# A fused attention and two-expert kernel: the experts' steps start four slots later beside the attention, and the opening is reordered

## The chip, the cores and the metric

The kernel runs on 1 core of a Trainium2 chip. The metric is the device time of one execution in microseconds (us); lower is better. The kernel before takes 1138.91 us (median of 3 runs, 1137.67 to 1141.26).

Five engines run their own instruction lists in order and meet only at semaphores: PE (TensorE, matrix products and transposes), DVE (VectorE), ACT (ScalarE), POOL (GpSimd), and SP (SyncE), which here only issues DMAs. "An engine waits" means that its next instruction stands at a semaphore and everything behind it stands too.

## The reference, cut to what matters

```python
# attention: B=4, H=8, S=768, D=40; state is D x D for each (b, h)
for t in range(S):
    y[:, :, t] = einsum('bhd,bhde->bhe', r_t, state)
    Sa = einsum('bhde,bhe->bhd', state, a_t)
    state = state * w_t[..., None, :] - Sa (x) b_t + v_t (x) k_t
x = y as rows: 3072 tokens x 320
# first expert: d_ff 1024
h = ((x @ w1) * (x @ w2)) @ w3
x2 = h @ w_out
# second expert: d_ff 2048
out = maximum(x2 @ w_in, 0)**2 @ w_out2
```

Everything is float32. The products of the experts are taken from operands split into a rounded part and its rest ("hi" and "lo"), three products for each.

## The kernel before, in words

**Attention.** The sequence is cut into chunks of 64 tokens; a *window* n is one chunk of half of the batch, 24 windows in all (`WINDOWS`), windows with even n for one half of the batch and odd n for the other. A window is a chain of small steps over all engines: `turn_w`, `turn_ar`, `turn_bk` (transposes of loaded rows, PE), `scan` (running decay, DVE), `cross` (PE), `mask_ak` and `fill_lanes` (DVE), `invert` (POOL: 62 dependent operations that invert a 32x32 triangular block in all lanes at once), `turn_inverse` (DVE: brings the inverse into place), `make_u0`, `make_x1`, `make_u1`, `turn_uv`, `add_state`, `make_read`, `make_y`, `turn_state` (PE), with copies on ACT between them. At the end `scale_y` (DVE) writes y, `store_y` (SP) stores it to DRAM (`xT`).

**Experts.** The tokens are cut into 6 *tiles* (`TILES`) of 512, and tile i needs the y of windows 4i to 4i+3: `load_x` (SP) brings them back from DRAM, `round_x` (ACT) makes `xT_hi`, `rest_x` (DVE) makes `xT_lo`. A tile is 56 *steps* (each a `yield` of the generator `experts()` that every engine has): steps 0 to 23 are the first expert (a_f and b_f, products of 8 matmuls into `aside`, L848, and `fold`, L901), steps 24 to 55 are the second (c_f, L848, alternating with `project`, L916, here called p_f). `round_x` of the next tile stands in step 54 on ACT, `rest_x` in step 54 on DVE; steps 52 to 55 are c15, p13, p14, p15.

**Folding and splitting.** w3 and w_out of the first expert are multiplied once, in 8 parts (`turn_w3`, `multiply_w3` on PE, `round_fold` on ACT, `rest_of_fold` on DVE, `store_fold` on SP into `fold_rows`). The other weights are split into hi and lo once: the raw weights are loaded into one of 3 `stage` buffers (`load_staged`), `round_split` and `rest_of_split` make the parts in a slot of `w_ring` or `v_ring`, `pass_split` on SP stores them and issues the load of the split three further on. These splits stand beside tile 0, each in a step of its own (`slot_of_w`, `due`), those below zero before it.

**Order.** It is written out by hand, the same on each engine. First the *opening*: windows 0 to 3 whole, the first part of window 4 (up to `make_z(4)`), the first part of window 5 (up to `cross(5)`), the folding, and splits 0 to 2. Then the *loop*: for n from 4 to 23, 14 slots a window; in each slot every engine does a piece of window n (or n+1, n+2) and then `next(beside)`, one step of the experts. So windows 4 to 23 stand beside 280 steps, that is tiles 0 to 4, and tile 5 (56 steps) runs alone after the attention. Before, step t stands in slot t: the 14 slots of window 4 have steps 0 to 13, and each tile begins with the first slot of window 8, 12, 16 or 20. On PE the slots of window n are, in order: `turn_ar(n+1)` s0, `make_z(n)` s1, `turn_bk(n+1)` s2, `cross(n+1)` s3, s4, `make_u0(n)` s5, `turn_rows(n+1)` s6, `make_x1(n)` s7, `turn_w(n+2)` `make_u1(n)` s8, `turn_uv(n)` s9, `add_state(n)` s10, `make_read(n)` s11, `make_y(n)` s12, `turn_state(n)` s13, where s0 to s13 are the expert steps. For n = 4 the first four of these attention pieces are left out on PE, since the opening has done them. `turn_ar(n+1)` waits for `st_copied`, which is `copy_state` on ACT, and that stands on ACT behind step s12.

Of the kernel before, what the change touches and what calls it, by code (L numbers as in the profile page):

```python
# [5 lines left out]
F32 = mybir.dt.float32  # L6
# [71 lines left out]
def attention_with_experts(nc, xT_dram, inputs, w1, w2, w3, w_out, w_in, w_out2, out):  # L78
# [8 lines left out]
    T, M = out.shape  # L87
# [4 lines left out]
    DX = M + REM  # L92
    FT, FT2 = F // P, F2 // P
# [5 lines left out]
    W_FIRST, V_FIRST = FT + FT2 // 2, FT + FT2  # L99

    OPENING = 4
    LEAD = 0
    LOOK = 3
    assert REM * 2 == P and TOK == B * 2 * C and STAGE >= 2 * DX

# [8 lines left out]
    with ExitStack() as ctx:  # L114
# [94 lines left out]
        def wait(eng, s, value):  # L209
            if value > 0:  # L210
                eng.wait_ge(s, value)
# [74 lines left out]
        def turning(u):  # L286
            return banks[2 + u % 2]

        def folding(ft):
            return banks[4 + ft % 2][:, 0:M]  # L290


        def slot_of_w(at):
            return max(3 * at - 7, -1) if at < FT else 19 if at == FT else 17 + 4 * (at - FT)

        splits = sorted([(slot_of_w(at), 0, at) for at in range(W_FIRST)] +
                        [(23 + 2 * f, 1, FT + f) for f in range(FT2)])
# [6 lines left out]
        for x in range(FT + len(splits)):  # L304
            before = staged_count[x - LOOK] if x >= LOOK else 0
            staged_count.append(before + 16 * (1 if x < FT or splits[x - FT][1] else 6))

        def wait_fold_stored(eng):
            for x in range(RING):
                eng.wait_ge(fold_stored[x], 64 * len(range(x, FT, RING)))  # L310


        clears = [azk[0], rbd[0], azk[1], rbd[1], *spare, *zv, *sT, *st]
# [20 lines left out]
        def _(sp):  # L334
            def begin(loads):
                for signal, buffer, src in loads:
                    sp.dma_start(buffer, src).then_inc(signal, 16)
# [25 lines left out]
            def load_wo():  # L363
                for h in range(2):
                    rows = w_out[GT // 2 * P * h:GT // 2 * P * (h + 1), :].rearrange("(t p) m -> p t m", p=P)
                    sp.dma_start(wo_raw[h][:].rearrange("p (t m) -> p t m", m=M), rows).then_inc(loaded_wo, 16)
# [18 lines left out]

            def store_fold(ft):
                sp.wait_ge(fold_split, ft + 1)
                for rest, t in enumerate((h_hi, h_lo)):
                    row, src = fold_rows[ft][:, DX * rest:DX * (rest + 1)], t[ft % RING][:, 0:M].bitcast(F32)
                    sp.dma_start(row[:, 0:M], src).then_inc(fold_stored[ft % RING], 16)  # L390
                    sp.dma_start(row[:, M:DX], src[:, 2 * P:M]).then_inc(fold_stored[ft % RING], 16)

# [30 lines left out]
            def load_v(at):  # L423
                x = at % V_FIRST
                if x < FT:
                    sp.wait_ge(fold_stored[x % RING], 64 * (x // RING + 1))
                if V_FIRST <= at < V_FIRST + SLOTS:
                    sp.wait_ge(v_stored[at % SLOTS], 16 * (FT2 // SLOTS))
                wait(sp, h_used, at - SLOTS + 1)
                dst = v_ring[at % SLOTS][:].bitcast(F32)  # L430
                if x < FT:
                    sp.dma_start(dst, fold_rows[x]).then_inc(v_loaded[at % SLOTS], 16)
                else:
                    sp.dma_start(dst[:, 0:2 * M], wout_rows[x - FT]).then_inc(v_loaded[at % SLOTS], 16)
# [3 lines left out]
            def pass_split(x):  # L438
                store_split(x)
                if x + LOOK < len(splits):  # L440
                    load_staged(FT + x + LOOK)
# [5 lines left out]
                    yield  # L447

            def experts():
                w_at = v_at = SLOTS  # L450
                for i in range(TILES):
                    for f in range(FT + LAG):
                        if f < FT:
                            yield
                            if W_FIRST <= w_at < W_LOADS:
                                load_w(w_at)
                            w_at += 1
                            yield
                        if f >= LAG:
                            if v_at < FT or V_FIRST <= v_at < V_LOADS:  # L460
                                load_v(v_at)
                            v_at += 1
                            yield
                    for f in range(FT2 + LAG):
                        if f < FT2:
                            if f % 2:
                                if W_FIRST <= w_at < W_LOADS:
                                    load_w(w_at)
                                w_at += 1
                            yield  # L470
                        if f >= LAG:
                            if v_at < FT or V_FIRST <= v_at < V_LOADS:
                                load_v(v_at)
                            v_at += 1
                            if f < FT2 + LAG - 1:
                                yield
                    wait_drained(sp, f"o{SUB - 1}", i)
                    wait_drained(sp, f"o{SUB - 2}", i)
                    wait_drained(sp, "o0", i)
                    wait_drained(sp, "o1", i)  # L480
                    sp.dma_start(out.rearrange("(b s) m -> s b m", b=B)[2 * C * i:2 * C * (i + 1)],
                                 out_rows[:]).then_inc(out_stored, 16)
                    yield

            beside = split_first()
            def next_w(n):
                sp.wait_ge(turned_w, n)
                begin(inputs.w_loads(n))

            def next_ar(n):  # L490
                sp.wait_ge(turned_ar, n)
                begin(inputs.ar_loads(n))

            def next_bk(n):
                sp.wait_ge(turned_bk, n)
                begin(inputs.bk_loads(n))
# [14 lines left out]
            begin(inputs.ar_loads(0))  # L511
            begin(inputs.bk_loads(0))
            load_staged(0)
            begin(inputs.uv_loads(0))
            next_w(1)
            load_wo()
            next_ar(1)
            load_staged(1)
            next_bk(1)
            sp.wait_ge(cleared, len(clears))  # L520
            begin(inputs.zv_loads(0))
            begin(inputs.zv_loads(1))
            next_w(2)
            load_staged(2)
            next_ar(2)
            begin(inputs.uv_loads(1))
# [31 lines left out]
            next_zv(5)  # L558
            store_fold(5)
            store_y(2)  # L560
            load_x(0, 0)
            store_y(3)
            load_x(0, 1)
            pass_split(0)
            store_fold(6)
            next_staged(10)
            pass_split(1)
            load_v(0)
            load_v(1)
            store_fold(7)  # L570
            load_v(2)
            load_v(3)
            pass_split(2)
            next_uv(5)
            beside = split_first()
            for n in range(OPENING, WINDOWS):
                one, two = window_steps(n)
# [87 lines left out]
        def _(pe):  # L665
# [255 lines left out]
                last.then_inc(h_used, 1)  # L921

            def experts():
                pe.wait_ge(y_scaled, OPENING)
                pe.wait_ge(st_copied, OPENING)
                for i in range(TILES):
# [37 lines left out]
            cross(0)  # L964
            turn_w(1)
            turn_rows(0)
            multiply_w3(0, 0)
            make_z(0)
            turn_ar(1)
            multiply_w3(0, 1)  # L970
            multiply_w3(0, 2)
            turn_bk(1)
# [135 lines left out]
        def _(act):  # L1108
# [66 lines left out]
            def round_fold(ft):  # L1175
                act.wait_ge(multiplied, ft + 1)
                wait(act, fold_stored[ft % RING], 64 * (ft // RING))
                nc.scalar.copy(h_hi[ft % RING][:, 0:M], folding(ft)).then_inc(fold_rounded, 1)

            def round_split(x):  # L1180
                _, kind, at = splits[x]
# [8 lines left out]
            def round_hidden(x, i):  # L1190
                at = (FT + FT2) * i + x
                wait_made(act, x, i)
                if at == 0:
                    wait_fold_stored(act)
                wait(act, h_used, at + 1 - RING)
                nc.scalar.copy(h_hi[at % RING][:], hidden[x % 2][:]).then_inc(hi_made, 1)  # L1196

# [16 lines left out]
                nc.scalar.copy(xT_hi[:], x_raw[:]).then_inc(x_rounded, 1)  # L1214

            def experts():
                act.wait_ge(multiplied, FT)
                for i in range(TILES):
                    for f in range(FT + LAG):
# [106 lines left out]
            copy_w3(7)  # L1326
            round_x(0)
            round_fold(7)
            round_split(2)
            for n in range(OPENING, WINDOWS):  # L1330
                one, two = window_steps(n)
                if OPENING < n and one:
# [32 lines left out]
        def _(dve):  # L1365
# [97 lines left out]

            def rest_of_fold(ft):
                dve.wait_ge(fold_rounded, ft + 1)
                nc.vector.tensor_tensor(h_lo[ft % RING][:, 0:M], folding(ft), h_hi[ft % RING][:, 0:M].bitcast(F32),
                                        ALU.subtract).then_inc(fold_split, 1)

            def rest_of_split(x):
# [34 lines left out]
                nc.vector.tensor_tensor(xT_lo[:], x_raw[:], xT_hi[:].bitcast(F32), ALU.subtract).then_inc(x_split, 1)  # L1504

            def experts():
                for i in range(TILES):
                    for f in range(FT + LAG):
                        if f < FT:
# [89 lines left out]
            invert_decay(4, 0)  # L1599
            new_state(1)  # L1600
            scale_a(4)
            turn_inverse(2)
            invert_decay(4, 1)
            mask_read(1)
            scale_bk(4)
            rest_of_fold(4)
            scale_y(1)
            mask_ak(4)
# [3 lines left out]
            add_x1(2)  # L1612
            invert_decay(5, 1)
            rest_of_split(0)
            turn_inverse(3)
            rest_of_fold(5)
            new_state(2)
            rest_of_split(1)
            mask_read(2)
            add_x1(3)  # L1620
# [6 lines left out]
            scale_bk(5)  # L1627
            rest_x(0)
            rest_of_fold(7)
            rest_of_split(2)  # L1630
            for n in range(OPENING, WINDOWS):
                one, two = window_steps(n)
                if OPENING < n and one:
# [65 lines left out]
```

## Time and profile before

| | |
|---|---|
| median of 3 runs | 1138.91 us |
| profiled execution | 1141.75 us |
| its span (first to last instruction) | 1139.3 us |
| PE busy | 1065.8 us, 94% of the span |
| POOL, DVE, ACT busy | 559.7, 634.3, 411.3 us |
| mean granted TensorE clock | 0.969 of full |
| moved by DMA | 172.74 MB, mean 152 GB/s |

Span and execution differ by 2.45 us, which lie around the span. The page of the profile cuts the span into 40 slices of 28.5 us and gives the busy share of each engine in tenths, and the clock that TensorE was granted. An engine's idle time is listed before the instruction that ended it, with the releaser.

### The profile page before, as it was taken

How to read it: one execution, taken by the hardware profiler on the slowest of the kernel's cores; microseconds unless marked ns; L12 is line 12 of the kernel's file. 1: busy time of each engine (PE TensorE's matmuls, PEld its weight loads, DVE VectorE, ACT ScalarE, POOL GpSimd, SP SyncE). 2: the span in 40 equal slices, each digit the busy share in tenths (PEclk: the TensorE clock that was granted, in tenths of full speed). 3: DMA queues.
4: the chain of work that ended last, by engine and by line, in shares of the span. 5: the costliest groups of instructions: out<-in, count | busy, mean ns of one | idle time of the engine just before them, and what ended most of it. 6: DMA issues, size and time to landing. Idle time of an engine off the chain costs nothing.

```text
span 1139.3 us, 27869 instructions
## 1 busy us (share of the span) xinstructions
PE 1065.8 (94%) x11056; PEld 903.7 (79%) x11056; DVE 634.3 (56%) x987; ACT 411.3 (36%) x771; POOL 559.7 (49%) x1573
## 2 busy tenths in 40 slices
PE   4997879999979999989999998999998999988998
PEld 4776757888867888877888986888886888876897
DVE  5866336677745566646466655566565556332343
ACT  2443323444433244323244333234333234322232
POOL 5778707367554374573464672554662654700000
PEclk9998889999989999998999998999998999998999
DMA  9943277666866546655545656546555453454552
GB/s 182 178 91 79 62 218 204 149 179 201 225 189 150 147 132 162 155 159 139 153 129 149 146 167 149 146 131 151 149 162 145 139 153 120 127 167 160 167 173 81
DMA packets 269504, 172.74 MB, mean 152 GB/s; under 512 B 201792, under 2 KB 231488, under 8 KB 269376
## 3 DMA queue, kind: packets, MB, share of 16 engines
q1 hardware_dynamic: 269376, 170.97, 57.0%
q8 instruction: 88, 1.44, 0.5%
q14 instruction: 40, 0.33, 0.1%
HBM read 144.18 MB, written 26.74 MB: 150 GB/s over the span
## 4 chain that ended last, share of the span: by engine, by line
PE 74%; DVE 3%; DMA 2%; issue 2%; SPq 2%; ACT 1%; DVEq 0%; ACTq 0%
PE aside L848 30%; PE moe_bank L916 13%; PE moe_bank L901 9%; PE both L810 3%; PE both L711 3%; PE both L752 2%; PE both L744 2%; PE both L825 2%; PE both L821 2%; PE both L695 2%; PE both L793 2%; PE both L724 1%; PE both L705 1%; PE both L801 1%; PE both L775 1%
## 5 line engine op out<-in xcount | busy, mean ns | idle before, releaser
L650 POOL TENSOR_TENSOR inv_tmp<-blk,inv 128x60 f32<-128x60 f32 (+24 forms) x744 | 253.0, 340 | 261.1 <-DVE blk L1419 204.1
L654 POOL TENSOR_TENSOR inv<-inv,inv_tmp 128x60 f32<-128x60 f32 (+24 forms) x744 | 263.7, 354 | 58.2
L916 PE MATMUL moe_bank<-v_ring,h_hi 128*128 128x320 f32 x768 | 178.5, 320 | 0.0
L848 PE MATMUL aside<-xT_hi,w_ring 128*128 128x512 f32 x480 | 143.0, 430 | 16.7 <-DVE xT_lo L1504 7.2
L1499 DVE TENSOR_TENSOR hidden<-left 128x512 f32<-128x512 f32 x96 | 68.0, 708 | 129.6 <-ACT left L1208 129.6
L1196 ACT CAST h_hi<-hidden 128x512 fp32r<-128x512 f32 x144 | 89.5, 621 | 124.6 <-DVE hidden L1495 78.9
L848 PE MATMUL aside<-x2T_hi,w_ring 128*128 128x512 f32 x480 | 132.7, 406 | 0.0
L916 PEld LDWEIGHTS moe_bank<-v_ring,h_hi 128*128 128x128 f32 x768 | 127.3, 189 | 3.8
L1487 DVE TENSOR_TENSOR h_lo<-hidden,h_hi 128x512 fp32r<-128x512 f32 x144 | 99.3, 690 | 51.4 <-ACT h_hi L1196 50.6
L1208 ACT ACTIVATE left<-aside 128x512 f32<-128x512 f32 x96 | 57.3, 597 | 178.8 <-PE aside L848 113.0
L848 PEld LDWEIGHTS aside<-xT_hi,w_ring 128*128 128x128 f32 x480 | 90.5, 201 | 36.0 <-DVE xT_lo L1504 7.5
L916 PE MATMUL moe_bank<-v_ring,h_lo 128*128 128x320 f32 x384 | 119.0, 310 | 0.0
L848 PEld LDWEIGHTS aside<-x2T_hi,w_ring 128*128 128x128 f32 x480 | 84.0, 188 | 14.9 <-ACT x2T_hi L1232 0.2
L901 PE MATMUL moe_bank<-h_hi,v_ring 128*128 128x512 f32 x288 | 92.8, 403 | 0.0
L848 PE MATMUL aside<-xT_lo,w_ring 128*128 128x512 f32 x288 | 86.1, 409 | 0.0
L1377 DVE RECIPROCAL undecay<-decay 104x256 f32<-104x256 f32 x48 | 83.7, 1745 | 0.5
L848 PE MATMUL aside<-x2T_lo,w_ring 128*128 128x512 f32 x288 | 81.5, 391 | 0.0
L916 PEld LDWEIGHTS moe_bank<-v_ring,h_lo 128*128 128x128 f32 x384 | 72.5, 189 | 0.0
L1495 DVE TENSOR_TENSOR hidden<-left,aside 128x512 f32<-128x512 f32 x48 | 32.5, 676 | 69.7 <-PE aside L848 69.7
L848 PEld LDWEIGHTS aside<-xT_lo,w_ring 128*128 128x128 f32 x288 | 57.7, 200 | 13.4
L635 POOL MEMSET azk<- 64x512 f32 x20 | 10.4, 522 | 109.8 <-PE both L744 109.6
L848 PEld LDWEIGHTS aside<-x2T_lo,w_ring 128*128 128x128 f32 x288 | 54.1, 188 | 12.2 <-DVE x2T_lo L1521 0.2
(144 smaller groups left out, 1628.1 us busy)
## 6 DMA issues: line engine op xcount, KB each, us to landing
w_ring<-gate_rows SPq DMA_DIRECT2D x40, 640.0 KB, 4.0
w_ring<-win_rows SPq DMA_DIRECT2D x40, 640.0 KB, 4.0
v_ring<-wout_rows SPq DMA_DIRECT2D x80, 320.0 KB, 3.0
v_ring<-fold_rows SPq DMA_DIRECT2D x48, 384.0 KB, 3.3
gate_rows<-w_ring SPq DMA_DIRECT2D x8, 640.0 KB, 4.1
win_rows<-w_ring SPq DMA_DIRECT2D x8, 640.0 KB, 3.6
wout_rows<-v_ring SPq DMA_DIRECT2D x16, 320.0 KB, 3.4
stage<-in_moe_w SPq DMA_DIRECT2D x8, 512.0 KB, 4.8
```

Source lines behind the costliest of these rows:

```text
L650: nc.gpsimd.tensor_tensor(tmp, x[:, j, 0:j].unsqueeze(2).broadcast_to([P, j, X - lo]), mine[:, j:j + 1, lo:X].broadcast_to([P, j, X - lo]) ...
L654: nc.gpsimd.tensor_tensor(mine[:, 0:j, lo:X], mine[:, 0:j, lo:X], tmp, ALU.add).then_inc(solve, 1)
L711: last = nc.tensor.matmul(its_both(n)[:, x * P:(x + 1) * P], bkT[n % 2][0:E, x].rearrange("e z s -> e (z s)"), azk[n % 2][0:E, x].rearrang ...
L810: last = nc.tensor.matmul(its_both(n)[:, x * P:(x + 1) * P], uvT[0:E, x, :], rbd_of(n)[0:E, x].rearrange("e q t -> e (q t)"), start=True, ...
L848: last = nc.tensor.matmul(bank(use), w, x, start=n == 0, stop=n == len(terms) - 1)
L901: last = nc.tensor.matmul(bank(f"x{m}"), weights[:, lo:lo + P], h[at % RING][:], start=f == 0 and n == 0, stop=f == FT - 1 and n == 2)
L916: last = nc.tensor.matmul(bank(f"o{s}")[:, 0:M], h[at % RING][:, s * P:(s + 1) * P], weights[:, rest * M:(rest + 1) * M], start=f == 0 and ...
L1196: nc.scalar.copy(h_hi[at % RING][:], hidden[x % 2][:]).then_inc(hi_made, 1)
L1208: drain(nc.scalar.activation(left[x % 2][:], bank(use), ACT.Relu), use)
L1377: nc.vector.reciprocal(undecay[0:E, xs], decay[n % 4][0:E, xs, 1:C + 1]).then_inc(undecayed, 1)
L1487: nc.vector.tensor_tensor(h_lo[at % RING][:], hidden[x % 2][:], h_hi[at % RING][:].bitcast(F32), ALU.subtract).then_inc(lo_made, 1)
L1499: nc.vector.tensor_tensor(hidden[x % 2][:], left[x % 2][:], left[x % 2][:], ALU.mult).then_inc(squared, 1)
```

## The change

The constant `LEAD` goes from 0 to 4. Each engine's `experts()` yields four times before its first step, so step t stands in slot t+4: slots 0 to 3 of the loop (window 4) hold no expert step, each later tile begins in slot s4 of window 8, 12, 16 or 20, and 60 steps run after the attention. `due` subtracts `LEAD`, so splits keep their step. The split of a2's weights goes from the opening to step 0.

The opening is reordered on SP, PE and DVE, `turn_inverse(2)` and `turn_inverse(3)` stand later on DVE, and the parts 6 and 7 of the folding are rounded and split in slots 2 and 3 of `v_ring` and no longer in `h_hi`/`h_lo`, so the first roundings of the experts wait for the stores of parts 0 to 5 only, and `load_v(2)`, `load_v(3)` wait for the stores of 6 and 7.

```diff
-    LEAD = 0
+    LEAD = 4
...
+        def folded(ft, rest):
+            if ft < 2 * RING:
+                return (h_hi, h_lo)[rest][ft % RING][:, 0:M]
+            return v_ring[SLOTS - FT + ft][:, M * rest:M * (rest + 1)]
...
-            return max(3 * at - 7, -1) if at < FT else 19 if at == FT else 17 + 4 * (at - FT)
+            return max(3 * at - 7, -1 if at < 2 else 0) if at < FT else 19 if at == FT else 17 + 4 * (at - FT)
...   (SP, load_v)
+                if SLOTS - FT + 2 * RING <= at < SLOTS:
+                    ft = FT - SLOTS + at
+                    sp.wait_ge(fold_stored[ft % RING], 64 * (ft // RING + 1))
...   (experts() of SP, PE, ACT and DVE)
+                for _ in range(LEAD):
+                    yield
...   (SP, opening)
             load_staged(0)
-            begin(inputs.uv_loads(0))
             next_w(1)
-            load_wo()
-            next_ar(1)
-            load_staged(1)
-            next_bk(1)
             sp.wait_ge(cleared, len(clears))
             begin(inputs.zv_loads(0))
+            next_ar(1)
+            load_wo()
+            next_bk(1)
+            load_staged(1)
             begin(inputs.zv_loads(1))
             next_w(2)
+            begin(inputs.uv_loads(0))
             load_staged(2)
...
             store_y(2)
+            pass_split(0)
             load_x(0, 0)
+            pass_split(1)
             store_y(3)
             load_x(0, 1)
-            pass_split(0)
+            next_staged(10)
             store_fold(6)
-            next_staged(10)
-            pass_split(1)
             load_v(0)
             load_v(1)
             store_fold(7)
+            next_uv(5)
             load_v(2)
             load_v(3)
-            pass_split(2)
-            next_uv(5)
...   (PE, opening)
-            multiply_w3(0, 0)
             make_z(0)
             turn_ar(1)
+            multiply_w3(0, 0)
...   (ACT)
-                nc.scalar.copy(h_hi[ft % RING][:, 0:M], folding(ft)).then_inc(fold_rounded, 1)
+                nc.scalar.copy(folded(ft, 0), folding(ft)).then_inc(fold_rounded, 1)
...
-                if at == 0:
-                    wait_fold_stored(act)
+                if at < RING:
+                    act.wait_ge(fold_stored[at], 64 * 2)
...
             round_fold(7)
-            round_split(2)
...   (DVE, opening)
             scale_a(4)
-            turn_inverse(2)
             invert_decay(4, 1)
             mask_read(1)
             scale_bk(4)
+            turn_inverse(2)
             rest_of_fold(4)
...
             rest_of_split(0)
-            turn_inverse(3)
             rest_of_fold(5)
             new_state(2)
+            turn_inverse(3)
             rest_of_split(1)
...
             rest_of_fold(7)
-            rest_of_split(2)
```

`store_fold` and `rest_of_fold` use `folded` in the same way.

## Rows read from the trace of the kernel before

**Rows 1.** The page: busy us (share of the span) xinstructions of each engine.
```profile
PE 1065.8 (94%) x11056; PEld 903.7 (79%) x11056; DVE 634.3 (56%) x987; ACT 411.3 (36%) x771; POOL 559.7 (49%) x1573
```

**Rows 2.** Timeline (start us, us, what [idle before <- releaser]), PE after the tile seams.
```profile
339.26 1.92 PE L695 MATMUL both<-ident,ar_raw 128*104 128x128 f32 x8 [4.85 <-ACT st L1166]
...
531.71 1.43 PE L848 MATMUL aside<-xT_hi,w_ring 128*128 128x512 f32 x5 [0.52 <-DVE hidden L1495]
...
862.18 1.92 PE L695 MATMUL both<-ident,ar_raw 128*104 128x128 f32 x8 [4.79 <-ACT st L1166]
```

**Rows 3.** The chain in order of time (start us, us, what), seam before tile 2.
```profile
504.07 0.70 DVE y_out L1461
...
509.56 2.33 DMA x_raw<-xT
...
513.29 0.43 ACT st L1166
```

**Rows 4.** Windows: us; busy of PE, PEld, DVE, ACT, POOL; PEclk, DMA share, GB/s.
```profile
513.90:518.80 4.90, 4.90 (x16) 3.96 (x16) 4.87 (x6) 1.62 (x4) 0.00 (x0) 0.50 0.05 18
...
150.00:180.00 30.00, 21.84 (x100) 16.02 (x99) 12.72 (x20) 8.89 (x17) 5.59 (x17) 0.77 0.81 215
```

**Rows 5.** The chain: pieces at full clock, and the end of the attention.
```profile
202.72 0.87 PE both L695 x8
203.59 1.84 PE aside L848 x8
205.43 1.06 PE both L744 x32
...
211.48 1.79 PE both L711 x16
...
493.91 1.76 PE moe_bank L916 x12
...
1017.69 1.05 PE both L825 x32
```

**Rows 6.** Timeline of PE: start of tile 0, late tile 0, start of tile 5.
```profile
150.63 1.40 PE L848 MATMUL aside<-xT_hi,w_ring 128*128 128x512 f32 x5
...
180.12 0.76 PE L775 MATMUL both<-uv,n 32*32 32x40 f32 x32
...
317.01 1.51 PE L793 MATMUL both<-ident,uv 128*104 128x128 f32 x8 [2.77 <-DVE decay L1369]
...
1029.65 2.50 PE L848 MATMUL aside<-xT_hi,w_ring 128*128 128x512 f32 x5 [7.22 <-DVE xT_lo L1504]
```

**Rows 7.** Timeline of ACT at the start of tile 0.
```profile
156.66 0.83 ACT L1188 CAST w_ring<-stage 128x768 fp32r<-128x768 f32 x1 [5.41 <-DMA stage<-in_moe_w]
...
165.94 0.62 ACT L1196 CAST h_hi<-hidden 128x512 fp32r<-128x512 f32 x1 [7.97 <-DMA fold_rows<-h_lo]
```

**Rows 8.** Timeline of SP (start us, us of issuing, what), end of the opening.
```profile
127.31 1.57 SPq L346 DMA_DIRECT2D xT<-y_out  x4
...
139.23 1.95 SPq L346 DMA_DIRECT2D xT<-y_out  x4
...
144.65 0.59 SPq L403 DMA_DIRECT2D gate_rows<-w_ring  x1
```

**Rows 9.** Timeline of PE and POOL in the opening.
```profile
95.13 1.93 PE L821 MATMUL aside<-rbd,st 40*40 40x64 f32 x32 [5.96 <-DVE ruv L1453]
...
117.57 0.76 PE L752 MATMUL aside<-x_row,invT 32*32 32x40 f32 x32 [2.55 <-DVE invT L1425]
...
116.61 0.20 POOL L654 TENSOR_TENSOR inv<-inv,inv_tmp 128x8 f32<-128x8 f32 x1
```

**Rows 10.** Timeline: DVE from `mask_ak` to `fill_lanes`; POOL's first solve in the loop.
```profile
526.86 0.86 DVE L1406 COPY diag<-both 32x256 f32<-32x256 f32 x2 [1.81 <-PE both L711]
...
529.07 2.01 DVE L1419 STREAM_TRANSPOSE blk<-diag 128x1024 f32<-128x1024 f32 x1
...
173.16 0.25 POOL L650 TENSOR_TENSOR inv_tmp<-blk,inv 128x31 f32<-128x31 f32 x1 [30.31 <-DVE blk L1419]
```

More of the change, by code:

```diff
@@ L306, in attention_with_experts @@
             staged_count.append(before + 16 * (1 if x < FT or splits[x - FT][1] else 6))
-        def wait_fold_stored(eng):
-            for x in range(RING):
-                eng.wait_ge(fold_stored[x], 64 * len(range(x, FT, RING)))
         clears = [azk[0], rbd[0], azk[1], rbd[1], *spare, *zv, *sT, *st]
@@ L387, in store_fold @@
                 sp.wait_ge(fold_split, ft + 1)
-                for rest, t in enumerate((h_hi, h_lo)):
-                    row, src = fold_rows[ft][:, DX * rest:DX * (rest + 1)], t[ft % RING][:, 0:M].bitcast(F32)
+                for rest in range(2):
+                    row, src = fold_rows[ft][:, DX * rest:DX * (rest + 1)], folded(ft, rest).bitcast(F32)
                     sp.dma_start(row[:, 0:M], src).then_inc(fold_stored[ft % RING], 16)
@@ L923, in experts @@
             def experts():
+                for _ in range(LEAD):
+                    yield
                 pe.wait_ge(y_scaled, OPENING)
@@ L1216, in experts @@
             def experts():
+                for _ in range(LEAD):
+                    yield
                 act.wait_ge(multiplied, FT)
@@ L1465, in rest_of_fold @@
                 dve.wait_ge(fold_rounded, ft + 1)
-                nc.vector.tensor_tensor(h_lo[ft % RING][:, 0:M], folding(ft), h_hi[ft % RING][:, 0:M].bitcast(F32),
+                nc.vector.tensor_tensor(folded(ft, 1), folding(ft), folded(ft, 0).bitcast(F32),
                                         ALU.subtract).then_inc(fold_split, 1)
@@ L1506, in experts @@
             def experts():
+                for _ in range(LEAD):
+                    yield
                 for i in range(TILES):
```

## The prediction

> **What bounds the kernel now.** I read the page first: PE is busy for 1065.8 of 1139.3 us and the next engine for little more than half of the span [rows 1]. So no engine but PE is a bound over the whole, and a change can gain only what PE stands idle (73.5 us) and what it loses at the lower clock. No product is taken away. Then I listed PE's idle times in order of time. They lie in four places: the opening, the start of tile 0, once at each tile seam, and before tile 5. Between two seams, 174 us apart (862.18 less 339.26, by three [rows 2]), PE has hardly a gap, so what the change does to the steady part is worth nothing unless it makes new gaps.
>
> A seam, in the chain of waits [rows 3]: the last `make_y` before it ends, `scale_y` starts at 504.07, y goes to DRAM and comes back as x_raw at 511.89, 7.8 us after `make_y`. ACT stands at `round_x` in step 54 for all that time, since step 54 is the very slot in which y is made. Behind it stands `copy_state`, which ends at 513.72, and `turn_ar` on PE waits for that: 4.85 us idle at the first seam, 4.79 at the last of four [rows 2]. After the gap PE gets half the clock (granted 0.50, that is 1.2 of 2.4 GHz) for 4.9 us [rows 4], so it loses another 2.4. Each seam costs 7.3 us. Before tile 5 the same trip costs 7.22 idle [rows 6], and a slow stretch of the same kind after it, 2.4: 9.6.
>
> The start of tile 0: from the first a0 at 150.63 to the end of `fold(0)` at 180.12 [rows 6]. In it are six products into `aside` at 1.84 (11.0), one `fold` (9 matmuls for 8: 2.1), `make_u0` and `turn_rows`, which I set at the 0.87 of `turn_ar` (1.7) [rows 5]: 14.8 us of work in 29.5. So 14.7 are lost, to two waits of ACT [rows 7], 5.41 for the raw weights of split 2 and 7.97 for the stores of fold parts 6 and 7, which the buffers of the first rounded hidden rows share, and to the clock (0.77 in the mean over these 30 us [rows 4]).
>
> **The change part by part.**
>
> *Four slots of lead, at the seams.* It adds and removes no instruction. `round_x` of the next tile moves from slot s12 to s2 of the next window. Counted on PE from the end of `make_y` with the pieces of [rows 5]: c14 1.84, `turn_state` (as `turn_ar`) 0.87, p12 1.76, `turn_ar` 0.87, c15 1.84, `make_z` 1.06: 8.2, after which ACT has a copy and a rounding before `round_x`, which it reaches at some 9 (estimate), and x is there at 7.8. `copy_state` and `turn_ar` are now ahead of it in ACT's list. The first a0 comes after p13, `turn_bk` (as `turn_ar`), p14, `cross` 1.79 and p15 more, at 16.2; `xT_lo` is ready at about 9 + 3.1 = 12.1 (tile 5 starts 10.9 after the end of the last `make_y` [rows 5, 6]; less the trip's 7.8 that leaves 3.1 for the two roundings). So 4 us of cover are left, and the seam is free: 4 x 7.3 = 29.2. The price below that: should x come 4 us later than now, a0 waits, no longer `turn_ar`. In each tile a wait of 0.52 for `combine`, queued behind `fill_lanes` on DVE [rows 2, 10], falls in slots where a1 and b1 stood; b1 now stands in s7, away from `fill_lanes` (s3): four of these, 2.0 less, and I count 1.5.
>
> *Before tile 5.* Behind the last `make_y` (ends 1018.74) two steps stood; now six: 2 x 1.84 + 4 x 1.76 = 10.7. The trip to `xT_lo` ends 10.9 after `make_y` [rows 5, 6]. Of 9.6 us 0.3 stay: 9.3 gained. The four steps that are now alone after the attention cost what they cost beside it, since both take PE in turn.
>
> *The uncovered slots 0 to 3.* On PE they hold nothing for window 4, so nothing is exposed there but `make_u0(4)`, which stood behind five steps and now stands behind one. It waits for `mask_ak(5)`; DVE gets there only after `rest_of_fold(7)`, whose product ends just before a0 starts at 150.6 (some 1.2 us for ACT's and DVE's part), `turn_inverse(4)` (0.7, both estimates) and 2.2 us of masking (526.86 to 529.07 [rows 10]): 154.7, and a0 from 150.6 ends at 152.5. So 2.2 us of idle. Below it: 0, if a0 itself is later; above: 6, if ACT's `copy_blocks(5)` is late too. POOL's inversion of window 5, which waited 30.3 us until 173.16 [rows 10], starts some 16 us sooner and is no bound.
>
> *The two waits at the start of tile 0.* The load for split 2 now goes out ahead of `store_fold(6)` and stands in no engine's way until step 0; the first rounding waits for parts 0 and 3 only, stored long before. Both waits go (above: one of them stays with 3 us). What is late next is x itself. SP has 10.3 us free between `store_y(2)` and `store_y(3)` (128.9 to 139.2 [rows 8]); into it go `load_x(0,0)` (four issues as `store_y`'s, 2.0 [rows 8]) and now two `pass_split`, each 7 issues of 0.59 (4.1) [rows 8]: 10.2, and waits between them, so `store_y(3)` goes out 0.2 to 1 us later, and I give a0 2 us of delay in all, with a slow stretch of 2.4 behind it. With the wait at `make_u0(4)`, partly inside it, 6 us of loss stay: 14.7 - 6 = 8.7 gained (3 to 13).
>
> Here a rule of the Trainium skill speaks against the change: "DMA: Bandwidth & Descriptors", section "Two DMAs through the same engine are not ordered", says that within one queue of one engine descriptors start in order, so y(3) would stand behind the 1.28 MB that the second `pass_split` has just sent. No run here shows that yet. At the 215 GB/s of [rows 4] these last 6.0 us, most of which have gone by when y(3) is issued: 1.5 us more by the rule, none without it. Both are inside the term's bounds.
>
> *The opening's order.* `zv_loads(0)` ahead of 1.8 MB lets `make_z(0)` go up to 5 us sooner; DVE's `turn_inverse(2)` no longer holds `mask_read(1)`, which takes away 5.96 us at 95.13; the slow 1.93 beside it goes too [rows 9]. But `make_u0(3)` at 117.57 waits for the inverse, and POOL, which does one solve after the other, ends that one at 116.81 [rows 9]. POOL's first solve starts from `fill_lanes(0)`, whose loads and predecessors are not touched. So all that PE wins before goes into a longer wait there. Behind it I count 1 us, for `new_state(2)` ahead of `turn_inverse(3)` (below: 2 us lost by a longer slow stretch after a longer gap; above: 4, if that slow stretch gets shorter).
>
> *Late in tile 0* PE waits 2.77 at 317.01 [rows 6], and runs slowly after it, as a split's load came late from an SP queue full with window 7's transfers. This burst now meets an earlier step, when loads of 6 DMAs still go out. Between 4 us gained and 6 lost I take 0.
>
> The sum: 29.2 + 1.5 + 9.3 + 8.7 + 1.0 + 0 = 49.7. Against it I set 3.5 us for waits that no row shows: the steps of the first expert meet the attention's pieces in another phase in each tile. That leaves 46.2. Against the profiled execution (span 1139.3, and 2.45 around it, 1141.75) this is 1095.6; the median of the runs shown is 2.84 lower, 1138.91, so I forecast 1093 for it. My own range for this case is 1081 to 1104.
>
> **The rivals.**
>
> 1. *The seam wait stays in part.* If ACT meets `round_x` before x, or DVE's `rest_x` in front of `mask_ak` holds `make_u0`, a gap of about half stays at each seam, with the slow stretch whole: 2.5 gained for 7.3. 4 x 4.8 = 19 less: 1112. For it: ACT's margin is under 1 us by my count. Against: `turn_ar` no longer depends on it, and a0 has 4 us.
>
> 2. *SP decides.* The passes ahead of `store_y(3)` and the burst in window 7 cost a full gap each, with its slow stretch: 10 us less, 1103. For it: SP's 10.3 us are filled to the brim, and the wait at 317.01. Against: y(3) needs only its own four issues.
>
> 3. *The lead buys nothing at the start.* The four slots are lost: PE stands for four steps of 1.84, and nothing of the 8.7 comes back: 16 less, 1109. For it: window 4's chain runs over four engines with a single step beside it. Against: PE has no piece in these slots.
>
> 4. *Slower.* DVE's block of `mask_ak` and `fill_lanes` (4.2 us, 526.86 to 531.08 [rows 10]) meets the hand-over from b to `fold` in both windows of each tile's first expert, in tiles 0 to 4: twice 4.2 and twice 2.4 of clock, 13.2 a tile, 66 in all: 1159. It turns the sign from 9.2 us a tile on. For it: the 0.52 us behind this very block in the old phase. Against: two more products stand between b and its `fold`, about 4 us, and the old phase has only that one gap.
>
> **How the numbers follow.** The forecast has 0.62, rival 1 0.12, rival 2 0.17, rival 3 0.06, rival 4 0.03. A measurement of this kernel tells 0.3% (3.4 us) from no change. All but rival 4 are faster by far; 0.01 I leave for no change: faster 0.96, same 0.01, slower 0.03. For 8 in 10 the range goes from 1081 (the forecast with the upper bounds of the opening, the start and tile 0) to 1112, where rival 1 lies.
>
> **What would show it.** At the four seams, in slot s0 of windows 8, 12, 16 and 20, no idle before L695 and the clock at 1.00; `round_x` on ACT after x's landing with at most 1 us of wait; before tile 5 less than 1 us. Before tile 0's first product 1 to 3 us for `xT_lo`, before `make_u0(4)` up to 2. PE idle before `make_u0(3)` grown from 2.55 to some 9, at the same time, 117. PE's idle sum down from 73.5 to about 42. The forecast is wrong if an idle of over 2 us stands in any seam, if the stretch from tile 0's first product to `fold(0)` takes over 24 us, or if the steps of the first expert in tiles 1 to 4 show new gaps of together more than 4 us.

## The result and the profile after

The changed kernel takes 1100.67 us (median of 4, 1100.09 to 1102.29); the kernel before in the same comparison 1139.24. The ratio is 0.9663 (95% interval 0.9644 to 0.9681): 3.4% faster. The forecast was 1093 (1081 to 1112): 46 us were to go, 38.6 went. By the total alone this lies nearer to rival 2's 1103 than to the forecast, so only the traces can say which parts came true. In two later comparisons (*changed_again* and *changed_third* below) the ratio was 0.9631 (0.9595 to 0.9666) and 0.9641 (0.9626 to 0.9655).

The profiled execution took 1100.62 us with a span of 1098.1, 41.2 less than in the profile before (that execution took 1141.75, more than the median, so the two spans differ by more than the two medians). The page after, busy time (answering to [rows 1]) and granted clock in 40 slices:

```profile
PE 1052.2 (96%) x11056; PEld 895.0 (81%) x11056; DVE 634.2 (58%) x987; ACT 415.1 (38%) x771; POOL 553.1 (50%) x1573
...
PEclk9999699999999999999999999999999999999999
```

PE stands idle for 45.9 us, not 73.5: 27.6 less. And it is busy for 13.6 us less with the same 11056 products: that is the clock, 0.969 in the mean before, 0.984 after. From the sixth slice on the row shows no drop, but in the fifth there is a deeper one than anywhere before.

**The seams.** PE and ACT where tile 2 begins, timeline, answering to [rows 2, 3]:

```profile
492.89 1.03 PE L701 MATMUL both<-ident,ar_raw 128*104 128x128 f32 x8
...
504.82 1.32 PE L854 MATMUL aside<-xT_hi,w_ring 128*128 128x512 f32 x5
...
491.15 0.43 ACT L1174 COPY st<-both 104x320 f32<-104x320 f32 x1
...
497.81 1.48 ACT L1222 CAST xT_hi<-x_raw 128x1536 fp32r<-128x1536 f32 x1
...
500.85 1.75 DVE L1513 TENSOR_TENSOR xT_lo<-x_raw,xT_hi 128x1536 fp32r<-128x1536 f32 x1
```

No row has an idle in brackets. `copy_state` (L1174) is done before `turn_ar`, and `round_x` (L1222) starts without a wait, at once after ACT's own work; `xT_lo` is ready at 502.6, 2.2 us ahead of a0. From 309 us to the end no idle time of PE over 0.4 us is left, at any seam or inside a tile; the four waits of 0.52 are gone too. Tile 5 starts at 990.67 without one, answering to 7.22 us of [rows 6].

**The opening and the start of tile 0,** PE's timeline, answering to [rows 6, 9]:

```profile
118.21 1.28 PE L758 MATMUL aside<-x_row,invT 32*32 32x40 f32 x32 [8.85 <-DVE invT L1434]
...
154.59 1.40 PE L854 MATMUL aside<-xT_hi,w_ring 128*128 128x512 f32 x5
...
158.95 0.76 PE L758 MATMUL both<-x_row,invT 32*32 32x40 f32 x32 [2.28 <-DVE azk L1419]
```

and the clock behind that gap, in windows (busy of PE, PEld, DVE, ACT, POOL; clock, DMA share, GB/s), in the changed kernel and, second fence, in the kernel before:

```profile
118.20:134.00 15.80, 15.68 (x226) 14.35 (x226) 3.84 (x6) 3.70 (x8) 12.62 (x40) 0.50 0.21 65
```

```profile
118.50:126.40 7.90, 7.71 (x112) 7.18 (x112) 3.69 (x6) 1.62 (x4) 6.41 (x20) 0.57 0.35 81
```

The first product of tile 0 comes at 154.59, 4.0 us later than before, though nothing was added ahead of it: PE now runs 15.8 us at half clock behind `make_u0(3)`, not under 8. After that the start of tile 0 has 2.6 us of idle left (2.28, and 0.34 at `make_u1(4)`), where 14.7 were lost. From its first product to the start of `fold(0)` it takes 19.6 us, to the end of it 21.7.

**Late in tile 0,** a place that got worse, with its longest wait; PE, ACT and SP, timeline, answering to the 2.77 us of [rows 6]:

```profile
308.96 1.92 PE L799 MATMUL both<-ident,uv 128*104 128x128 f32 x8 [5.20 <-DVE decay L1378]
...
304.68 0.83 ACT L1196 CAST w_ring<-stage 128x768 fp32r<-128x768 f32 x1 [4.86 <-DMA stage<-in_moe_w_in]
...
296.14 0.47 SPq L383 DMA_DIRECT2D stage<-in_moe_w_in  x1
```

ACT waits 4.86 us for the raw weights of the last w split. SP issued them from 296.14 to 300.93, behind window 7's ar, zv, x and bk loads. `scan` stands on DVE behind that split, and `turn_uv(7)` waits for `scan`. But this wait is only half of what got worse here: it grew from 2.77 to 5.20, by 2.4. Another 2.8 us are idle at places where PE did not wait in the kernel before, above all before `make_z(6)` (0.60) and `cross(7)`, PE's timeline:

```profile
242.08 2.42 PE L717 MATMUL both<-azk,bkT 104*128 104x128 f32 x16 [1.68 <-DVE bkT L1407]
```

There `scale_bk` (DVE, L1407) starts at 240.81, behind 1.7 us of work on the rests of two splits, though `turn_bk` is done at 238.6. *lead_alone* has the same two gaps (0.60 and 1.70), so they come with the lead; no run here takes them away.

The account of the 41.2 us, from both traces: seams and tile 5, idle 19.7 + 2.1 + 7.2, clock 12.0: 41.0. Start of tile 0: 12.1. Opening: -4.0. Late tile 0: idle 4.8 before, 10.0 after, and some 1.7 more by the clock: -6.9. Sum 42.2, 1.0 more than the spans differ. The 2.4 us of clock at each seam and at tile 5 are those of [rows 4], taken for all five.

### The profile page after: what moved, and what is told of

Read it like the earlier page. It is cut to its first block, busy times and chain, and to the rows that moved or that the text cites. A ratio compares the mean times of both kernels' runs of the same rounds, so it can differ in the third digit from the quotient of the medians.

```text
span 1098.1 us, 27872 instructions
## 1 busy us (share of the span) xinstructions
PE 1052.2 (96%) x11056; PEld 895.0 (81%) x11056; DVE 634.2 (58%) x987; ACT 415.1 (38%) x771; POOL 553.1 (50%) x1573
## 4 chain that ended last, share of the span: by engine, by line
PE 77%; DVE 3%; issue 2%; SPq 2%; ACT 1%; DMA 0%; DVEq 0%; ACTq 0%
PE aside L854 30%; PE moe_bank L922 15%; PE moe_bank L907 9%; PE both L816 3%; PE both L717 3%; PE both L758 2%; PE both L750 2%; PE both L831 2%; PE both L827 2%; PE both L799 2%; PE both L701 1%; PE both L730 1%; PE both L840 1%; PE both L781 1%; PE both L807 1%
## 5 line engine op out<-in xcount | busy, mean ns | idle before, releaser
L656 POOL TENSOR_TENSOR inv_tmp<-blk,inv 128x60 f32<-128x60 f32 (+24 forms) x744 | 244.4, 328 | 252.2 <-DVE blk L1428 195.2
L854 PE MATMUL aside<-xT_hi,w_ring 128*128 128x512 f32 x480 | 132.8, 406 | 0.1
L854 PEld LDWEIGHTS aside<-xT_hi,w_ring 128*128 128x128 f32 x480 | 84.5, 188 | 16.6 <-DVE xT_lo L1513 0.3
L854 PE MATMUL aside<-xT_lo,w_ring 128*128 128x512 f32 x288 | 81.5, 391 | 0.0
L854 PEld LDWEIGHTS aside<-xT_lo,w_ring 128*128 128x128 f32 x288 | 54.1, 188 | 11.9
L1151 ACT COPY uv<-both 32x320 f32<-32x320 f32 x88 | 36.7, 417 | 62.2 <-PE both L758 60.8
```

Of the source, the lines that this page charges most:

```text
L656: nc.gpsimd.tensor_tensor(tmp, x[:, j, 0:j].unsqueeze(2).broadcast_to([P, j, X - lo]), mine[:, j:j + 1, lo:X].broadcast_to([P, j, X - lo]) ...
L854: last = nc.tensor.matmul(bank(use), w, x, start=n == 0, stop=n == len(terms) - 1)
L1151: last = nc.scalar.copy(uv[n % 2][rows, :, q, 0:D], by_head(its_first(n), rows))
```

## The experiments

Twelve runs were made: ten edited kernels, and the changed kernel twice more. All ratios are against the kernel before on the same chip; where two variants are compared in us, both ran there.

**1. The lead alone, the opening's edits alone.**

```diff
(the kernel before)
-    LEAD = 0
+    LEAD = 4
...   (experts() of the four engines)
+                for _ in range(LEAD):
+                    yield
```

> The kernel before with nothing but the lead of four slots. Theory (the seams and the start of tile 5 are the lead's own gain, 41 us by the trace of before, and the late part of tile 0 loses some 7): 1105 us (1098 to 1112), no idle over 0.5 us at the four seams, the two ACT waits at the start of tile 0 (5.4 and 8.0 us) still there in about their size. Rival (the lead pays only together with the new opening, since the four uncovered slots then expose the waits at the start of tile 0): 1120 us or more.

Measured: 1106.12 us where the kernel before took 1143.33, ratio 0.9673 (0.9632 to 0.9714). No seam has an idle time over 0.4 us, nor has tile 5. Its start of tile 0, PE's timeline and ACT's:

```profile
150.93 1.40 PE L850 MATMUL aside<-xT_hi,w_ring 128*128 128x512 f32 x5 [0.91 <-DVE xT_lo L1510]
...
161.24 1.27 PE L754 MATMUL both<-x_row,invT 32*32 32x40 f32 x32 [8.22 <-DVE azk L1416]
...
155.98 0.83 ACT L1192 CAST w_ring<-stage 128x768 fp32r<-128x768 f32 x1 [5.50 <-DMA stage<-in_moe_w]
```

The wait for split 2's weights is there in its old size (5.50) and now stands before `make_u0(4)`. The wait for the fold stores (7.97 before) no longer shows, against the expectation: the first rounding comes later. The late part of tile 0 is as bad as in the changed kernel (4.61 us before `turn_uv(7)`). So nearly the whole gain is the lead's.

```diff
(the changed kernel)
-    LEAD = 4
+    LEAD = 0
```

> The changed kernel with the lead set back to 0, so only the opening's edits are left. Theory (the opening before the first expert product loses 4 us to a longer slow stretch of TensorE's clock, the two waits behind it go and give back 10 to 12): 1132 us (1127 to 1137), the seams as in the kernel before, 7.3 us each. Rival (the opening's edits only serve the lead): 1139 us, within 0.3% of before.

Measured: 1138.96 us against 1143.33, ratio 0.9952 (0.9928 to 0.9976). My theory gave 0.994, the rival 1.000; the ratio lies by the theory, but the parts do not: the first product of tile 0 came at 157.46 (150.63 in the profile of the kernel before, from the first comparison), behind a gap of 9.9 us before `make_u0(3)`. The opening lost more and the waits behind it gave back more than I wrote.

**2. Half the lead.**

```diff
(the changed kernel)
-    LEAD = 4
+    LEAD = 2
```

> The changed kernel with a lead of two slots. Theory (the x trip of 10.9 us from the last make_y to xT_lo must be covered by PE's pieces: at a seam the two steps and the attention's pieces between still cover it nearly, before tile 5 only 7.1 us of steps stand): seams with at most 1 us idle, before tile 5 some 3.8 us idle and a slow stretch: 1107 us (1104 to 1111). Rival (each slot of lead takes back its share of every seam, so half of 29 us return, and half of 9): 1120 us.

Measured: 1118.03 us, ratio 0.9773 (0.9733 to 0.9813), that is 1113 on the scale of the first comparison: neither of the two, by 6 to 7 us from either. Seam before tile 2, ACT and PE, and PE before tile 5:

```profile
502.28 1.48 ACT L1222 CAST xT_hi<-x_raw 128x1536 fp32r<-128x1536 f32 x1 [2.00 <-DMA x_raw<-xT]
...
504.23 1.05 PE L711 MATMUL both<-ident,bk_raw 128*104 128x128 f32 x8 [0.50 <-ACT x_row L1145]
...
508.26 2.05 PE L717 MATMUL both<-azk,bkT 104*128 104x128 f32 x16 [0.55 <-DVE bkT L1407]
...
1005.76 2.50 PE L854 MATMUL aside<-xT_hi,w_ring 128*128 128x512 f32 x5 [4.58 <-DVE xT_lo L1513]
```

The counting of PE's pieces was right for the x trip: ACT waits 2.0 us at `round_x`, and a0 is late by 0.3. What I left out is what stands behind the waiting instruction: `copy_x`, then DVE's `rest_x` ahead of `scale_bk`. These let PE stand at three to five places of each seam, 1.5 to 2.4 us in all, 4.58 before tile 5, and in tile 0 `turn_uv` waits for `scan` in three windows.

**3. Is it the clock behind the gap?** 18 and then 9 extra products go into the gap; they are no part of the computation and their result is not read.

```diff
             add_state(2)
+            for _ in range(18):        # gap_nine: 9
+                nc.tensor.matmul(its_second(3), ident[:], wo_raw[0][:, 0:512], start=True, stop=True)
             make_u0(3)
```

> The changed kernel with 18 extra products (128x128 by 128x512, their result is not used) on PE in the idle time of 8.85 us before make_u0(3). Theory (the 16 us at half clock that follow that gap are its consequence, and cost 8 us against 3.4 in the kernel before): the slow stretch shrinks to under 4 us, the first expert product comes 5 to 8 us sooner, 1094 us (1091 to 1097). Rival (PE is held there by the hand-overs to ACT and DVE in window 2 and 3, whatever the clock): 1100 to 1102 us.

Measured: 1103.86 us, ratio 0.9656 (0.9608 to 0.9703): no gain. But the 18 products took 15.7 us and `make_u0(3)` came at 124.85, 6.6 late; from there to the first product of tile 0 it took 31.7 us and not 36.4, at full clock and with 1.3 us of wait for x in it. The total spoke for the rival, the trace for the theory, so a second run had half as many.

> As gap_filled, with 9 extra products in place of 18: at the 0.87 us that one took there they fill 7.9 of the 8.85 us before make_u0(3) and no longer delay it. Theory (clock): no stretch at half clock behind make_u0(3), the first expert product 5 to 7 us sooner than in the changed kernel, total 5 to 7 us below it. Rival (hand-overs hold PE there): total within 2 us of it.

Measured: 1095.9 us; the changed kernel beside it (*changed_again*) 1100.53. The clock in the same stretch, windows:

```profile
118.20:134.00 15.80, 14.67 (x312) 12.85 (x312) 5.91 (x10) 6.05 (x12) 12.73 (x40) 1.00 0.33 96
```

312 products for 226 in the same 15.8 us; the first of tile 0 at 149.84, 4.75 us before the 154.59 of the first profile. And with a gap of 8.8 to 9.9 us left open, PE is at half clock until 134 to 136 us in all four profiles that have it (changed kernel, *changed_third*, *opening_alone*, *lead_two*); with the gap filled, in neither of two. So the slow stretch is what the opening lost. The total fell by 4.6 and not by 5 to 7, and the intervals of the two ratios overlap (0.9561 to 0.9629 here); the next run shows a reason why the total tells less than the trace.

> The changed kernel itself, as the measure for the three beside it on this chip: 0.966 of the kernel before, 1098 to 1106 us. No theory differs on it.

1100.53 us (1095.08 to 1104.42), ratio 0.9631 (0.9595 to 0.9666). In its profile PE was slow elsewhere, 68.9 to 83, before the wait, and only shortly behind it. Windows:

```profile
68.90:83.00 14.10, 14.02 (x210) 11.11 (x210) 5.03 (x7) 1.95 (x4) 11.20 (x38) 0.54 0.34 91
118.00:134.00 16.00, 15.15 (x302) 13.61 (x303) 4.85 (x8) 6.05 (x12) 12.80 (x41) 0.84 0.30 91
```

That slow stretch cost nothing: PE came later to `make_u0(3)`, waited 5.37 us in place of 8.85, and got its clock back at about 122.5. First product of tile 0: 151.87. The kernel is the same, and by where the clock falls its opening ends 2.7 us sooner here than in the first profile. Its five runs spread over 9 us; but so do nine of the kernel before on that chip (1137.95 to 1148.63), so the spread is not the change's doing. *gap_nine* gains 2.0 us of opening against this profile and 4.75 against the first.

**4. Is `turn_inverse(2)` better where it is now?**

```diff
(DVE, the changed kernel)
             scale_a(4)
+            turn_inverse(2)
             invert_decay(4, 1)
             mask_read(1)
             scale_bk(4)
-            turn_inverse(2)
```

> The changed kernel with turn_inverse(2) back at its old place on DVE, so PE stands at 90 again as before and reaches make_u0(3) late. Theory (POOL's third solve sets make_u0(3) at 118 in either order, so moving turn_inverse(2) only shifts PE's idle time; what differs is the slow stretch behind make_u0(3), shorter after a shorter gap): make_u0(3) at 117 to 119, the gap before it under 4 us, total 0 to 5 us below the changed kernel. Rival (the move is worth the 6 us that it takes away at 95): total 4 to 6 us above it.

Measured: 1096.85 us (1093.33 to 1103.57), ratio 0.9619 (0.9588 to 0.9650), beside *changed_third*:

> The changed kernel once more, as the measure for the three beside it on this chip: 0.963 to 0.967 of the kernel before.

1101.54 us, ratio 0.9641 (0.9626 to 0.9655). The intervals overlap, so no gain is proved, but the rival's 4 to 6 us above the changed kernel are refuted. PE's timeline of inverse_back:

```profile
96.14 1.93 PE L827 MATMUL aside<-rbd,st 40*40 40x64 f32 x32 [6.34 <-DVE ruv L1462]
...
118.95 0.76 PE L758 MATMUL aside<-x_row,invT 32*32 32x40 f32 x32 [2.48 <-DVE invT L1434]
```

The gap of 6.34 is back, and `make_u0(3)` stands at 118.95, as in changed_third (118.94, behind a gap of 9.88). POOL sets that time: its solve ends at 118.19 and 118.18. The move only carries PE's idle time from 95 to 118.

**5. Using the gap.** The last pieces of window 2, which need no inverse of window 3, go ahead of the wait:

```diff
(PE)
             add_state(2)
-            make_u0(3)
             make_read(2)
-            make_x1(3)
             make_y(2)
             turn_state(2)
+            make_u0(3)
+            make_x1(3)
             make_u1(3)
...   (ACT: place_state(2), copy_state(2) ahead of copy_u(3, 0, ...);
...    DVE: mask_read(2), rest_of_split(1), scale_y(2) ahead of turn_inverse(3))
```

> The changed kernel with make_read(2), make_y(2), turn_state(2) ahead of make_u0(3) on PE, and what they need ahead of turn_inverse(3) and copy_u(3, 0) on DVE and ACT. Theory (POOL's third solve ends at 117 whatever PE does, so the 5 us of window 2's last pieces are free in its shade, and the shorter gap leaves a shorter slow stretch): first expert product 7 to 11 us sooner, total 6 to 10 us below the changed kernel. Rival (the end of the opening is set by the trip of window 3's y to x and back, whose start does not move): 0 to 3 us.

Measured: 1095.15 us (1094.31 to 1096.14), ratio 0.9586 (0.9558 to 0.9615), 5.4 below the changed kernel beside it, with intervals that overlap a little; first product at 149.37, 5.2 us sooner than in the first profile (7 to 11 were expected). Less than the 6 to 10 of the theory, more than the rival's: the chain of window 3 (`make_u0`, copy, `make_x1`, `add_x1`, `make_u1`) now lies bare with waits of 0.94 and 1.10, and a gap of 3.5 us and a slow stretch remain.

**6. The gap late in tile 0.**

```diff
-            ... 19 if at == FT else 17 + 4 * (at - FT)
+            ... 19 if at == FT else 17 + 4 * (at - FT) + 2 * (at == W_FIRST - 1)
```

> The changed kernel with the last split of a w slot in step 47 in place of 45, its load issued two steps later and used two steps later. Theory (the 5.2 us gap of PE at 309 is ACT waiting for this one load of six DMAs, queued on SP behind window 7's burst): the gap falls under 2 us, total 3 to 7 us below the changed kernel. Rival (DVE's load of splits beside the scan makes the gap): the gap stays at 4 to 6 us, total within 1 us.

Measured: 1095.96 us, ratio 0.9592 (0.9563 to 0.9621), 4.6 below the changed kernel; again the intervals overlap, and the trace has to tell. PE and ACT:

```profile
305.02 1.05 PE L799 MATMUL both<-ident,uv 128*104 128x128 f32 x8 [1.81 <-DVE decay L1378]
...
302.29 0.46 ACT L1193 CAST v_ring<-stage 128x320 fp32r<-128x320 f32 x1 [3.02 <-DMA stage<-in_moe_w_out]
```

The w split no longer waits; the next load in SP's queue does, for 3.02, and PE for 1.81 of 5.20. The edit moves the split's work on DVE too, so the run alone does not part the two theories; the trace of the changed kernel does. DVE stands idle there for 4.55 us, for ACT's rounded weights, right before the rest of the split:

```profile
305.54 0.69 DVE L1488 TENSOR_TENSOR w_ring<-stage,w_ring 128x512 fp32r<-128x512 f32 x1 [4.55 <-ACT w_ring L1196]
```

So it was SP's order, not DVE's load.

**7. Together.** both_mended is 5 and 6 in one; both_x also loads window 7's first half of x 12 slots later:

```diff
-                if n % 4 == 3:
+                if n % 4 == 3 and n > 7:
                     load_x(n // 4, 0)
...
+                if n == 7:
+                    load_x(1, 0)
                 if n % 4 == 3:
                     load_x(n // 4, 1)
```

> read_first and split_later together. Theory (two separate losses, one in the opening, one late in tile 0): both gains add, 7 to 11 us below the changed kernel, about 1091 us. Rival (what one gives is taken by the other's wait further on): no better than the better of the two, 4 to 5 us.

> both_mended with window 7's first half of x loaded beside the second half, 12 slots later, so that SP's burst in that window has four issues less. Theory (SP's queue is what is late there): the rest of the gap at make_u1/turn_uv of window 7 (1.8 us in split_later) falls under 1 us, 1 to 2 us below both_mended, the seam stays free since x has 4 us of cover. Rival (the 2.2 us of issues now ahead of the second half make x late and a0 of tile 1 waits): 0 to 2 us above both_mended.

Measured: 1089.84 us, ratio 0.9548 (0.9531 to 0.9565), and 1088.24 us, ratio 0.9534 (0.9519 to 0.9548); changed_third, on the same chip, 1101.54. They are 11.7 and 13.3 us below it, with intervals well clear of its 0.9626 to 0.9655, so the two edits together are a proved gain, and the gains add (5.4 and 4.6 alone). In both_x the wait for `scan` in window 7 is gone; what is left there, PE's timeline, and behind it the page's busy time:

```profile
303.04 1.13 PE L818 MATMUL both<-rbd,uvT 104*128 104x128 f32 x8 [0.65 <-DVE state_tmp L1453]
```

```profile
PE 1049.3 (97%) x11056; PEld 891.9 (82%) x11056; DVE 634.1 (58%) x987; ACT 415.0 (38%) x771; POOL 555.6 (51%) x1573
```

The step from both_mended to both_x (1.6 us) is within their intervals; its seams have no idle. both_x beats both the kernel before and the changed one.

## Why the prediction was right, point by point

- **The seams (29.2, and 1.5 for `combine`).** Right in mechanism and size: 19.7 + 2.1 us of idle and 9.6 of clock (2.4 at each seam) are gone, 31.4. lead_alone shows that it is the lead. The cover was 2.2 us and not 4: `round_x` began 0.5 us later than worked out, and on DVE `scale_bk` stood ahead of `rest_x` and held it 1.6 us, which I had forgotten.
- **Before tile 5 (9.3).** Right: 9.6. In gap_filled, where x took 8.1 us, PE waited 1.18 us there; the cover is nil, as counted.
- **Slots 0 to 3 and the two waits at the start of tile 0 (8.7, with 3 to 13).** Right in kind, better in size: 12.1. `make_u0(4)` waits 2.28 as worked out (2.2). x does not make a0 late, only because the opening ends late itself: `xT_lo` is ready at 154.33, a0 starts at 154.59. Where the opening is quicker x shows: 0.9 us in gap_nine, 1.2 in changed_again, 2.3 in inverse_back.
- **The rule of order within a queue cost nothing.** The rows of SP, kernel before and changed kernel: in both the load of x, which waits until the stores have landed, starts 1.26 us after the last store of y(3) is issued (141.18 to 142.44, and 144.94 to 146.20).

```profile
142.44 0.89 SPq L359 DMA_DIRECT2D x_raw<-xT  x2
```

```profile
143.20 1.74 SPq L348 DMA_DIRECT2D xT<-y_out  x4
146.20 0.90 SPq L361 DMA_DIRECT2D x_raw<-xT  x2
```

  The 1.5 us that I had set beside the rule of the Trainium skill ("DMA: Bandwidth & Descriptors", section "Two DMAs through the same engine are not ordered") are not there; whether the descriptors start in order these rows cannot show.
- **The opening (+1, with -2 to +4).** Wrong by 5 us and outside its bounds: -4.0. The step that failed is "all that PE wins before goes into a longer wait there": it does, but the middle of the term gave the slow stretch behind that wait nothing more, and the lower bound 2 us. It lasted 15.8 us and not 7.9, and by the granted clocks (0.50 and 0.57) cost 7.9 us and not 3.4, 4.5 more. `make_u0(3)` itself came 0.6 us later. gap_nine shows it, and read_first bears it out.
- **Late in tile 0 (0, with -6 to +4).** Mis-sized, and outside its bounds: -6.9. The burst was named, with the right queue and the right kind of load; I had no reason for the middle of the bounds, as there were 6 DMAs to add to a queue that was already late. split_later gives 4.6 back. The 2.8 us of new small waits, at `cross(7)` above all, were not in the term; they are of the kind that the next one was set aside for.
- **Waits that no row shows (-3.5).** In tiles 1 to 5 none came: they have no idle over 0.4 us. Those of tile 0 are counted in the line above. Rival 4 is refuted, as no `fold` waits. Rivals 1 and 3 are refuted; rival 2 held by half, in window 7 and not at `store_y(3)`, which SP issued 0.03 us after `scale_y(3)` ended, as before.
- **The signs.** None of the three that would have shown the forecast wrong is there: no idle at a seam, 21.7 us from the first product to the end of `fold(0)` where over 24 was the sign, and 0.2 us of new idle in each of tiles 1 to 4. The sum of PE's idle time is 45.9 where 42 was expected.

Sum: 46.2 forecast, 41.2 between the two spans. The two terms that failed are 11.9 us together; the others turned out better by 7.9 in all, 3.4 of it at the start of tile 0 and 3.5 by the reserve, and 1.0 is the error of my account. That the total came so near owes much to luck: the reserve had been set aside for other waits, and the start of tile 0 lost less partly because the opening ended late and left x the time it needed. The mechanism of the lead, 41.0 us in the account, needed none.

## What to carry to other kernels

Where an engine waits for a round trip through DRAM, count the other engine's pieces between the last producer and the first consumer and shift the streams against each other by that many; it cost no instruction and gave 3.3% where the local reordering alone gave 0.5%. Shift far enough for what is queued behind the waiting instruction, not only for the consumer itself (half the lead: 2.3% in place of 3.4 to 3.7%). And where one engine sets a time (POOL here), an earlier arrival of another there is worth nothing, and can be less than nothing if it lets that engine's clock fall: put independent work into the gap. To leave the idle time where it was may do as well (inverse_back, 4.7 us in the medians, not proved).

## What the runs showed of the hardware

- The slow stretch behind a gap has no fixed length. After 5 us idle at a seam, with transposes and products into `aside` following, it was 4.9 us at the clock of 1.2 GHz [rows 4]; after 8.85 us idle, with the attention's small products following, 15.8 us; after 5.37 us idle and the same products, about 4.5.
- Neither the pieces behind the gap nor its length settle it alone: in three profiles of the changed opening the same pieces follow the wait at 69 us. After 3.73 us idle PE was slow until about 73 (granted 0.55 from 69.2 on), after 2.65 us (split_later) and 3.07 us (changed_again) until about 82. What decides it no run here shows.
- A slow stretch where PE has slack costs nothing, and shortens the idle time behind it (68.9 to 83 in changed_again, 5.37 us idle then in place of 8.85).
- A float32 product of 128x128 by 512 took 0.87 us (15.7 us for 18).
- The trip of y to x, from the end of `scale_y` to the start of `xT_hi` at tile 5, differs from run to run: 6.9 us in the trace of the kernel before; 7.8, 7.9 and 8.1 in those of opening_alone, lead_two and gap_filled. It is not the chip alone: lead_alone ran on the same chip as these three and had x within 7.0 us.
